# First tile of a decay attention with two mixture layers behind it: who makes the decay powers and the mask, and when the second tile's scores are issued

## What is computed

```python
Dmask = np.where(rel >= 0, lam[:, None, None] ** rel[None, :, :], 0.0)
lam_pow = lam[:, None, None] ** (pos[None, :, None] + 1)
for b in range(nb):
    intra = np.einsum('bhic,bhjc->bhij', qb, kb) * Dmask[None]
    intra = np.einsum('bhij,bhjd->bhid', intra, vb)
    inter = np.einsum('bhid,bhde->bhie', qb * lam_pow[None], kv_state)
    out[:, :, sl] = intra + inter
    kv_state = lam_block * kv_state + np.einsum('bhsd,bhse->bhde', kb_dec, vb)
...
logits = x @ w_gate
...
h = np.maximum(xe @ w1[e], 0.0); ye = h @ w2[e]
...
g = h - np.tanh(h); return g @ w_out
```

## Time and profile before

| | us |
|---|---|
| median of three executions | 529.34 (528.69 to 530.26) |
| the profiled execution, its own time | 529.97 |
| its span in the trace | 528.2 |
| TensorE busy within the span | 510.6 |

### The profile page before, as it was taken

How to read it: one execution, slowest core, us unless ns; L and a number is a source line. 1 busy time by engine, 2 the same in 40 slices (tenths; PEclk the granted TensorE clock), 3 DMA queues, 4 the chain that set the end, 5 groups by cost and what they waited for, 6 DMA issues and landing times.

```text
span 528.2 us, 11152 instructions
## 1 busy us (share of the span) xinstructions
PE 510.6 (97%) x4001; PEld 455.4 (86%) x4002; DVE 361.3 (68%) x546; ACT 263.4 (50%) x486; POOL 317.9 (60%) x261
## 2 busy tenths in 40 slices
PE   5999989999999999999999999999999999999994
PEld 4899889999999999999888888888888888888883
DVE  7455555744544536455499999979987766997781
ACT  1344526765666656666455554545443444443431
POOL 4866147645545455455589898968754454865543
PEclk9999989999999999999999999999999999999998
DMA  8787548767777777784530000001100000100002
GB/s 312 279 282 262 190 138 259 244 201 238 201 232 237 192 235 215 218 237 143 193 129 0 2 1 1 0 1 40 40 2 0 1 0 1 60 22 1 0 1 79
DMA packets 32411, 64.57 MB, mean 122 GB/s; under 512 B 3696, under 2 KB 7792, under 8 KB 32368
## 3 DMA queue, kind: packets, MB, share of 16 engines
q1 hardware_dynamic: 30448, 57.71, 34.4%
q0 software_dynamic: 1920, 6.29, 3.5%
HBM read 57.69 MB, written 6.29 MB: 121 GB/s over the span
## 4 chain that ended last, share of the span: by engine, by line
PE 92%; DMA 2%; DVE 1%; POOL 1%; ACT 1%; issue 1%; SPq 0%; ACTq 0%
PE bank L325 27%; PE bank L327 27%; PE bank L326 27%; PE bank L1186 3%; PE bank L1161 2%; PE bank L1172 2%; PE bank L1207 1%; DMA qk_in<-in_qk_t_dram 1%; PE bank L352 1%; DMA x_sorted<-token_rows,tokid 1%; PE bank L1198 1%; PE bank L1214 1%; POOL w_l L626 0%; PE bank L1276 0%; PE bank L1371 0%
## 5 line engine op out<-in xcount | busy, mean ns | idle before, releaser
L626 POOL TENSOR_TENSOR w_l<-wst,w_h 128x512 fp32r<-128x512 f32 x64 | 86.9, 1359 | 78.9 <-ACT w_h L747 78.8
L675 POOL TENSOR_SCALAR big<-h_sq 128x512 uint8<-128x512 f32 x48 | 80.4, 1674 | 35.8 <-ACT h_sq L833 35.5
L689 POOL TENSOR_TENSOR g_l<-g,g_h 128x512 fp32r<-128x512 f32 x46 | 60.8, 1322 | 43.6 <-ACT g_h L843 43.6
L325 PE MATMUL bank<-wo_h,g_h 128*128 128x512 f32 x192 | 75.5, 393 | 0.1
L327 PE MATMUL bank<-wo_l,g_h 128*128 128x512 f32 x192 | 75.2, 391 | 0.0
L326 PE MATMUL bank<-wo_h,g_l 128*128 128x512 f32 x192 | 74.6, 389 | 0.0
L327 PE MATMUL bank<-x_l,win_h 128*128 128x512 f32 x188 | 74.3, 395 | 0.0
L325 PE MATMUL bank<-x_h,win_h 128*128 128x512 f32 x188 | 73.9, 393 | 0.0
L326 PE MATMUL bank<-x_h,win_l 128*128 128x512 f32 x188 | 73.7, 392 | 0.0
L325 PE MATMUL bank<-xs_h,w_h 128*128 (+1 forms) x256 | 70.8, 277 | 0.8 <-DVE xs_l L1055 0.8
L325 PE MATMUL bank<-h_h,w_h 128*128 128x232 f32 x256 | 70.3, 275 | 0.0
(11 more groups left out here) (153 smaller groups left out, 1109.0 us busy)
## 6 DMA issues: line engine op xcount, KB each, us to landing
wst<-in_w_dram SPq DMA_DIRECT2D x128, 256.0 KB, 2.9
qk_in<-in_qk_t_dram SPq DMA_DIRECT2D x12, 512.0 KB, 5.8
kv_in<-in_kv_dram SPq DMA_DIRECT2D x12, 512.0 KB, 4.7
win<-in_w_in_dram SPq DMA_DIRECT2D x8, 512.0 KB, 4.6
wo<-in_w_out_dram SPq DMA_DIRECT2D x8, 512.0 KB, 7.5
token_rows<-x_sb SPq DMA_DIRECT2D x12, 256.0 KB, 4.4
x_sorted<-token_rows,tokid POOLq DMA_INDIRECT x12, 4.1
out_dram<-rows,tokid POOLq DMA_INDIRECT x12, 3.1
```

The lines of the kernel that those rows point to most:

```text
L325: pe.matmul(dst, lh, rh, start=start, stop=False, skip_group_check=True)
L626: pool.tensor_tensor(w2_l[:, j % STG], wst2[:, j % STG], w2_h[:, j % 2].bitcast(F32), ALU.subtract).then_inc(w2l_ready, 1)
L675: pool.tensor_scalar(big[:, f % 2], h_sq[:, f % 2], T * T, None, ALU.is_ge).then_inc(big_ready, 1)
L689: pool.tensor_tensor(g_l[:, f % 2], g[:, f % 2], g_h[:, f % 2].bitcast(F32), ALU.subtract).then_inc(gl_ready, 1)
```

## The change

ScalarE makes the squares of the decay and the powers for q, ahead of `x_out(0)`; VectorE makes its half of `mask_blocks` with GpSimd waiting until the first half of the mask is complete; one load brings both layouts of the decay; `scores(1)` is issued in the middle of `outputs(0)`.

```diff
-        lam_sb = sb("lam_sb", [P, H], at=small_mem)
+        lam_sb = sb("lam_sb", [P, H + PAIRS], at=small_mem)
...
-            sp.dma_start(lam_sb[:], lam_all).then_inc(lam_in, 16)
+            sp.dma_start(lam_sb[:], lam_both).then_inc(lam_in, 16)
...
             load_qk(1)
-            sp.dma_start(lam_pair_sb[:], lam_pair).then_inc(lam_pair_in, 16)
             load_kv(1)
             sp.dma_start(w_gate_sb[:]...).then_inc(w_gate_in, 16)
...
             pool.wait_ge(near_step, 10)
+            pool.wait_ge(mask_ready, 1)
             mask_blocks(pool, head_halves[1]).then_inc(late_blocks_ready, 1)
...
             pool.wait_ge(mask_ready, 2)
             k_decayed(0)
-            pool.wait_ge(lam_pair_in, 16)
-            pool.tensor_copy(q_pow[:, :, 0:1], lam_pair_sb[:]...).then_inc(qpow_step, 1)
-            n = 1
-            while n < P:
-                pool.wait_ge(qpow_step, n.bit_length())
-                pool.tensor_tensor(q_pow[:, :, n:2 * n], q_pow[:, :, 0:n],
-                                   q_pow[:, :, n - 1:n].to_broadcast([P, PAIRS, n]), ALU.mult).then_inc(qpow_step, 1)
-                n *= 2
             k_decayed(1)
-            pool.wait_ge(qpow_step, POW_STEPS)
...
             pool.affine_select(out=tri[:], ...)
+            pool.wait_ge(qpow_step, POW_STEPS)
             for t in range(B, NT):
                 q_decayed(t)
...
         def _(act):
+            act.wait_ge(lam_in, 16)
+            for i in range(1, 7):
+                ge(act, lam_step, i - 1)
+                act.activation(lam_pow[:, i], lam_sb[:, 0:H] if i == 1 else lam_pow[:, i - 1],
+                               ACT.Square).then_inc(lam_step, 1)
+
+            act.copy(q_pow[:, :, 0:1], lam_sb[:, H:]...).then_inc(qpow_step, 1)
+            n = 1
+            while n < P:
+                act.wait_ge(qpow_step, n.bit_length())
+                for p in range(PAIRS):
+                    i = act.mul(q_pow[:, p, n:2 * n], q_pow[:, p, 0:n], q_pow[:, p, n - 1:n])
+                i.then_inc(qpow_step, 1)
+                n *= 2
...
             dve.wait_ge(lam_in, 16)
-            dve.tensor_tensor(lam_pow[:, 1], lam_sb[:], lam_sb[:], ALU.mult).then_inc(lam_step, 1)
...
-                if i + 2 < 7:
-                    square(i + 2)
...
                     if t == 0 and h == PAIRS:
+                        scores(1)
                         pe.wait_ge(sm_ready, 1)
...
             scores(0)
-            scores(1)
             pe.wait_ge(ident_ready, 1)
             pe.wait_ge(w_gate_in, 16)
```

More of the change, by code:

```diff
@@ L31, with decay_attention_moe_kernel @@
 POLY = (-0.019268172807322046, 2.644734663353291, -0.07151553627681556, 6.536064820179784)
-def decay_attention_moe_kernel(nc, qk_t, kv, lam_all, lam_pair, w_gate, w1, w2, w_in, w_out, out):
+def decay_attention_moe_kernel(nc, qk_t, kv, lam_both, w_gate, w1, w2, w_in, w_out, out):
     B, H, D = 2, 8, 64
@@ L142, in decay_attention_moe_kernel @@
         far_part = sb("far_part", [P, H, BLOCKS], at=small_mem)
-        lam_pair_sb = sb("lam_pair_sb", [P, PAIRS], at=small_mem)
         old = sb("old", [P, PAIRS, D], at=small_mem)
@@ L201, in decay_attention_moe_kernel @@
         lam_in = sem("lam_in")
-        lam_pair_in = sem("lam_pair_in")
         w_gate_in = sem("w_gate_in")
@@ L590, in _ @@
             k_decayed(0)
-            pool.wait_ge(lam_pair_in, 16)
-            pool.tensor_copy(q_pow[:, :, 0:1], lam_pair_sb[:].rearrange("p (a n) -> p a n", n=1)).then_inc(qpow_step, 1)
-            n = 1
-            while n < P:
-                pool.wait_ge(qpow_step, n.bit_length())
-                pool.tensor_tensor(q_pow[:, :, n:2 * n], q_pow[:, :, 0:n],
-                                   q_pow[:, :, n - 1:n].to_broadcast([P, PAIRS, n]), ALU.mult).then_inc(qpow_step, 1)
-                n *= 2
             k_decayed(1)
-            pool.wait_ge(qpow_step, POW_STEPS)
             pool.memset(ones[:], 1.0).then_inc(consts, 1)
@@ L698, in _ @@
         def _(act):
+            act.wait_ge(lam_in, 16)
[3 more added lines that the diff above has]
+                               ACT.Square).then_inc(lam_step, 1)
+            act.copy(q_pow[:, :, 0:1], lam_sb[:, H:].rearrange("p (a n) -> p a n", n=1)).then_inc(qpow_step, 1)
+            n = 1
[5 more added lines that the diff above has]
+                n *= 2
             def x_out(t):
@@ L884, in _ @@
             dve.wait_ge(lam_in, 16)
-            dve.tensor_tensor(lam_pow[:, 1], lam_sb[:], lam_sb[:], ALU.mult).then_inc(lam_step, 1)
             dve.wait_ge(seeds, 5)
-            def square(i):
-                dve.wait_ge(lam_step, i - 1)
-                dve.tensor_tensor(lam_pow[:, i], lam_pow[:, i - 1], lam_pow[:, i - 1], ALU.mult).then_inc(lam_step, 1)
             for i in range(5):
@@ L899, in _ @@
                     dve.wait_ge(near_step, 2 * i)
-                lam_n = lam_sb[:] if i == 0 else lam_pow[:, i]
+                lam_n = lam_sb[:, 0:H] if i == 0 else lam_pow[:, i]
                 dve.tensor_tensor(near_part[:, :, n:end], near[:, :, 0:end - n], every(lam_n, end - n),
                                   ALU.mult).then_inc(near_step, 1)
-                if i + 2 < 7:
-                    square(i + 2)
                 dve.wait_ge(near_step, 2 * i + 1)
@@ L1452 @@
         "kv": _np.concatenate([by_token(inputs["k"]), by_token(inputs["v"])], 2).reshape(ch * b, P, -1),
-        "lam_all": _np.broadcast_to(lam.reshape(pairs, 2).T.reshape(1, h), (P, h)),
-        "lam_pair": _np.repeat(lam.reshape(pairs, 2).T, d, axis=0),
+        "lam_both": _np.concatenate([_np.broadcast_to(lam.reshape(pairs, 2).T.reshape(1, h), (P, h)),
+                                     _np.repeat(lam.reshape(pairs, 2).T, d, axis=0)], 1),
         "w_gate": inputs["moe_w_gate"].reshape(kt, P, experts).transpose(1, 0, 2).reshape(P, -1),
```

## The result

The changed kernel takes 531.22 us (median of 20 executions, 528.61 to 533.25), the kernel before in 20 executions 530.12. The ratio is 1.0024, with a 95% interval of 1.0013 to 1.0036: 1.3 us slower by the ratio, between 0.7 and 1.9; the two medians alone differ by 1.1. The forecast was 530.6 us (529.1 to 532.0), that is +1.3 us and within 0.3% of before.

A forecast was written before the change was run, and what follows sets the result against it. TensorE, busy 510.6 of 528.2 us, was taken as the bound; its start waiting for the gate's weights gave +1.33 us, all other parts 0. Added to the 529.34 median: 530.6 us, range 529.1 to 532.0.

The forecast's parts named there:

- The wait that the diff leaves in place: Tile 0's first heads and `scores(1)` wait for the gate's weights, landing at 9.72; TensorE starts at 9.77 instead of 8.44.
- the removed small packets: Dropping one load's 128 small packets lets the gate's weights land 0.13 us earlier, bounds 0 and 0.47.
- The mask: VectorE's half alone takes 0.7 us; first masked scores at 8.35 instead of 10.12, hidden behind the weights' wait, worth 0.
- The powers for q: 28 multiplications on ScalarE ahead of `x_out(0)` take 7.0 us, from about 4.2 to 11.2; cost 0.
- The rival that they come late: ScalarE's powers end late, so `x_out(0)` starts at 14.1 to 15: +1.5 to +2.3 us, chance 0.04.
- Order and clock: Tile 0's TensorE products take 4.19 us as before, ending at 13.96; the clock's rise moves to 13.75.
- the rival of the late clock: TensorE's clock rises about 2 us later than forecast, at 15.8: +2.2 us, 531.5, chance 0.22.
- the sum: All parts together, with TensorE's start moved from 8.44 to 9.77: +1.33 us, the likeliest case, chance 0.37.
- distance that every later tile keeps: Tile 0's transposes come some 1.3 us later than 13.28, and every later tile stays that much later.
- the early clock: TensorE's clock rises at 12.4 as before although its work starts later: +0.6 us, chance 0.22.
- the wait costs nothing: The gate's weights are there by 8.4, so TensorE gains at most 0.1 us: no change, chance 0.10.

The follow-up runs named there:

- e1: Changed kernel with `scores(1)` issued ahead of the loop again, the rest of the change kept; ratio 0.9981 to the kernel before.
- e4: Changed kernel with the load of the gate's weights issued ahead of tile 1's q and k, the wait left in place; ratio 1.0003 to the kernel before.
- e3: Changed kernel with the wait for the gate's weights moved down to their first use, in tile 0's logits; ratio 1.0022 to the kernel before.
- g3: Changed kernel with the load of the gate's weights issued later, behind tile 2's q and k; ratio 1.0031 to the kernel before.
- e2: Kernel before with only `scores(1)` moved into the middle of tile 0's outputs; ratio 1.0024 to the kernel before.
- g1: f4 with 7 and 5 identity products ahead of and behind the first scores instead of 10 and 7; ratio 0.9957 to the kernel before.
- f1: Kernel before with identity products ahead of and behind `scores(0)`, keeping TensorE busy (warm); ratio 0.9978 to the kernel before.
- g2: The same kernel as e3, run once more; ratio 1.0033 to the kernel before.
- f4: e1 with identity products ahead of and behind `scores(0)`, keeping TensorE busy (warm); ratio 0.9961 to the kernel before.

## Why the prediction was right, point by point

**The wait that the diff leaves in place** is what delays the copy. The weights were put at 9.72 and landed at 9.80; TensorE started at 9.90, not 9.77, at the upper bound of the forecast. For the copy it is shown from four sides: undoing the order, moving the wait's load forward or moving the wait down each brings it back to 12.3 to 12.8 (e1, e4, e3), and moving the load back pushes it by 1.34 us (g3). e2 adds that a late mask does the same. That the loss of time goes with it is shown by e1 alone, whose interval lies apart from that of the changed kernel; those of e3, e4 and g3 do not. The value of the removed small packets was put at 0.13 us; the landing moved by 0.05 against the earlier trace rows. Since it came at 9.6 in e2 and at 10.06 in g1, no run shows this term.

**The mask.** Product on VectorE alone 0.7 at 6.2, measured 0.69 at 6.20; first masked scores 8.35, measured 8.45; second 10.3, measured 10.36. GpSimd's half took the expected 1.05. The 1.58 of the earlier trace rows was thus an effect of the two running side by side: f1, with the old arrangement, has 1.58 again. The Trainium skill, SBUF — State Buffer, section Who interferes with whom, says that a VectorE instruction with two inputs in SBUF contends with a GpSimd instruction that reads SBUF; the pair 1.58 and 0.69 agrees.

**The powers for q.** 7.0 us from 4.2 to 11.2 were forecast; they took 6.56 from 4.00 to 10.56, so ScalarE was free 3.57 us before its copy. The rival that they come late is ruled out. (The lower bound of 4.9 us was added up wrongly: with 0.11 between starts and 0.34 for a whole operation it is 28 x 0.11 + 7 x 0.23 + 0.42 = 5.1.) The Trainium skill, ScalarE: Activation LUTs, section What ACT_TABLE_LOAD costs, gives 186 ns and 0.83 ns per element, 93 ns more for a factor by pointer and 93 ns of overlap; worked out from it, an estimate of 28 x 0.186 + 7 x 0.093 + 508 x 0.00083 = 6.3 us, and the trace agrees within 5%.

**Order and clock.** The end of tile 0's products was put at 13.96, measured 14.08. Its clock rose later than the forecast 13.75 in the profiled execution, since `state_step(0)` at 13.87 is still at the lower level, so this execution lies between the sum and the rival of the late clock: its scores of tile 2 start 1.80 us later. At tile 2's copy it is 1.1 later (22.61 against 21.52), because the kernel before lost 0.57 us in a stall inside tile 2. The changed kernel has a stall of the same length inside tile 7, from 44.88 on, and from there it is 2.0 later (46.17 against 44.20). So the "distance that every later tile keeps" was not kept: it was 1.5, 1.8, 1.1 and 2.0 us, and 1.7 at the end of the span. What the stalls are the profile does not say; it names no releaser.

Over all executions the loss was 1.3, the sum. The mechanism was right, and so were the size and the sign; that the figure agrees to a tenth is luck. The interval is 1.2 us wide, the start was 0.13 later than forecast, and the clock's rise, which the sum took to move with the work, varies by more than that between executions of one kernel (e3 and g2 above). The rivals of the early clock (+0.6) and of the late clock (+2.2) lie just outside the interval.

**The rival "the wait costs nothing"** was worded as: even the best outcome of this change is no change. e4, where the weights are there early, has 1.0003, as it says. e1, e3 and e4 at equal clock are 0.5 to 0.7 us below the kernel before in their sessions, but by their ratios none is clear of 1, so a small gain is not excluded.

## What to carry to other kernels

When work is moved in an in-order program, list the waits that it is moved behind, and look up when each is released: a wait that was free because a longer piece of work covered it becomes the bound when that work moves to its far side. Put such a wait at the first use of what it guards, or the small load in front of the large ones. And before shortening a chain at the start of a kernel, see at which level of TensorE's clock the work beside it runs: here the faster mask was worth 0.9 us of start time only after the clock was brought up, and bringing it up took nothing but products in a gap, as long as they ended before the load that the next work waits for.

## What the runs showed of the hardware that was not expected

- The share of executions with a low mean granted clock depended on one idle gap 77 us into the kernel: 13 of 24 executions at 0.990 or less, and with five identity products in the gap 0 of 12. In profiled executions the granted clock fell to 0.50 shortly after gaps of 2.18 and 1.55 us (e3, e1), but not after one of 1.47 (g1). The warm kernels f1 to f4 had no such execution in 39, but the kernel before had only one in 26 in the same session, so that says nothing; g1 had one in 12.
- The rise of TensorE's clock at the start does not come at a fixed time in one kernel: in e3's two profiled executions the same 16 products took 0.63 us at 12.25 and 1.07 at 12.50. In the changed kernel they took 1.07 at 13.87, in g3, which began 1.4 us later, 0.63 at 15.25.
- The profile's granted clock reads 1.00 in the first microseconds, where the same products take 2.08 us instead of 1.16. The level there has to be read from durations.
- An identity product of 128 x 128 in fp32 takes 0.46 us at the lower level (10 in 4.64 us) and 0.26 us at the higher one (7 in 1.83 us).
- A stall of 0.57 us inside `outputs`, with no releaser named, sits in tile 2 in one kernel (20.29) and in tile 7 in the other (44.88), and shifts everything behind it.
